# Gate and value of a gated layer as 2x2 block products by Strassen's algorithm, in two sweeps over the tokens

## What is computed

```python
def _moe_ref(x, w_in, w_out):
    h = x @ w_in                                   # 2304 x 512 by 512 x 2048
    g = np.where(h > 0.0, h, np.exp(np.minimum(h, 0.0)) - 1.0)
    return g @ w_out                               # back to 512
...
def _moe2_ref(x, w_gate, w_val, w_out):
    g = x @ w_gate                                 # 512 x 1536
    silu = g * (1.0 / (1.0 + np.exp(-g)))
    val = x @ w_val                                # 512 x 1536
    return silu * val @ w_out                      # 1536 x 512
```

## Time and profile before

| | |
|---|---|
| median of 3 runs | 999.63 us (999.11 to 1001.42) |
| the profiled execution | 999.19 us, of which the span of the trace is 997.3 |
| TensorE busy | 985.8 us, 99% of the span, 7040 matmuls |
| VectorE, ScalarE, GpSimd busy | 46%, 34%, 12% |
| second layers on TensorE | from 542.87 us to the end |

### The profile page before, as it was taken

How to read it: one execution, slowest core, us unless ns; L and a number is a source line. 1 busy time by engine, 2 the same in 40 slices (tenths; PEclk the granted TensorE clock), 3 DMA queues, 4 the chain that set the end, 5 groups by cost and what they waited for, 6 DMA issues and landing times.

```text
span 997.3 us, 17826 instructions
## 1 busy us (share of the span) xinstructions
PE 985.8 (99%) x7040; PEld 912.5 (91%) x7040; DVE 455.7 (46%) x1151; ACT 341.0 (34%) x953; POOL 115.0 (12%) x138
## 2 busy tenths in 40 slices
PE   8899999999999999999999999999999999999998
PEld 5889999999999999999999888888888888889997
DVE  7888755556555565564343332223222322322222
ACT  5565544444435344443346321212121221212112
POOL 7204510023000000000057500000000000000000
PEclk9999999999999999999999999999999999999999
DMA  8544521124102111110434300200020001001000
GB/s 241 184 123 106 104 52 43 45 60 100 33 26 77 42 38 33 58 30 1 154 120 131 116 1 1 76 1 1 1 77 1 1 29 47 1 1 39 1 1 37
DMA packets 45666, 55.68 MB, mean 56 GB/s; under 512 B 6504, under 2 KB 33992, under 8 KB 45584
## 3 DMA queue, kind: packets, MB, share of 16 engines
q1 hardware_dynamic: 38128, 50.61, 16.5%
q0 software_dynamic: 6816, 3.55, 2.6%
q10 hardware_dynamic: 640, 0.39, 0.2%
HBM read 45.08 MB, written 9.44 MB: 55 GB/s over the span
## 4 chain that ended last, share of the span: by engine, by line
PE 95%; DVE 2%; ACT 2%; DMA 1%; issue 0%; ACTq 0%; POOL 0%; DVEq 0%; POOLq 0%
PE bank L455 29%; PE bank L457 28%; PE bank L456 28%; PE bank L419 2%; PE bank L386 2%; PE bank L404 1%; PE bank L441 1%; PE bank L395 1%; ACT weights L785 1%; DMA q_first<-qT 1%; DVE weights L616 1%; PE bank L429 0%; ACT prob L746 0%; DVE g_sb L641 0%; ACTq L360 0%
## 5 line engine op out<-in xcount | busy, mean ns | idle before, releaser
L455 PE MATMUL bank<-x_hl,weights 128*128 128x464 f32 (+3 forms) x928 | 325.8, 351 | 4.0 <-DVE weights L616 2.8
L457 PE MATMUL bank<-x_hl,weights 128*128 128x464 f32 (+3 forms) x928 | 322.0, 347 | 0.0
L456 PE MATMUL bank<-x_hl,weights 128*128 128x464 f32 (+3 forms) x928 | 321.9, 347 | 0.0
L455 PEld LDWEIGHTS bank<-x_hl,weights 128*128 128x128 f32 x928 | 175.5, 189 | 15.3 <-DVE weights L616 3.9
L456 PEld LDWEIGHTS bank<-x_hl,weights 128*128 128x128 f32 x928 | 175.6, 189 | 10.2
L457 PEld LDWEIGHTS bank<-x_hl,weights 128*128 128x128 f32 x928 | 175.5, 189 | 10.3
L455 PE MATMUL bank<-g_hl,weights 128*128 128x384 f32 (+1 forms) x448 | 147.7, 330 | 0.0
L457 PE MATMUL bank<-g_hl,weights 128*128 128x384 f32 (+1 forms) x448 | 143.3, 320 | 0.0
L456 PE MATMUL bank<-g_hl,weights 128*128 128x384 f32 (+1 forms) x448 | 143.2, 320 | 0.0
L659 DVE TENSOR_TENSOR u_sb<-bank,u_sb 128x464 f32<-128x464 f32 (+1 forms) x60 | 38.3, 638 | 202.3 <-ACT u_sb L807 202.3
L807 ACT ACTIVATE u_sb<-bank 128x464 f32<-128x464 f32 (+1 forms) x60 | 33.3, 555 | 196.4 <-PE bank L457 196.4
(11 more groups left out here) (96 smaller groups left out, 1062.5 us busy)
## 6 DMA issues: line engine op xcount, KB each, us to landing
landing<-w SPq DMA_DIRECT2D x44, 256.0 KB, 4.0
v_win<-v_windows SPq DMA_DIRECT2D x46, 105.0 KB
q_sb<-qT SPq DMA_DIRECT2D x88, 48.0 KB, 2.3
k_sb<-kT SPq DMA_DIRECT2D x14, 288.0 KB, 3.7
yT_scratch<-y_sb SPq DMA_DIRECT2D x20, 192.0 KB, 2.0
y_raw<-yT_scratch SPq DMA_DIRECT2D x4, 928.0 KB, 5.3
outT<-out_sb SPq DMA_DIRECT2D x16, 232.0 KB, 2.3
landing<-wg SPq DMA_DIRECT2D x12, 256.0 KB, 2.9
```

The costliest lines, as they stand in the source:

```text
L455: nc.tensor.matmul(out, w_hi, x_hi, start=first, stop=False)
L456: nc.tensor.matmul(out, w_hi, x_lo, start=False, stop=False)
L457: return nc.tensor.matmul(out, w_lo, x_hi, start=False, stop=last)
```

## The change

The gate matrix and the value matrix are each seen as 2x2 blocks: 256 input features by 128 hidden columns a block. The input is seen as blocks of 256 features by 256 tokens. For a pair of column blocks and 512 tokens, the four result blocks are made from seven block products instead of eight (the Winograd form), for gate and for value side by side in one bank (2 x 256 columns). The products are named p1, u2, u3, u4, c11, c21, c12. They need sums of weight blocks (`dve_sum_weights`, 4 operations for each matrix and pair), sums of input blocks (`dve_sum_blocks`, 4 for a tile), and seven sums of results on the way out of PSUM: a copy of p1 on ScalarE, and `dve_u2`, `dve_u3`, `dve_c22_u4` (two), `dve_c11`, `dve_c21`, `dve_c12` on VectorE. Seven blocks instead of four are split into high and low parts.

Since seven weight blocks with their low parts do not fit for all 12 column blocks, the hidden columns are done in two sweeps of three pairs. A sweep visits all tokens: one narrow tile of 256 tokens, done by plain block products, and four wide ones of 512; the second sweep goes backwards. The narrow tile is first and last. A visit and a pair are an item: 30 items. The first sweep's partial result goes to a scratch in HBM (`partT`), and comes back in the second, where VectorE adds it (`dve_out`). The second sweep's weights are loaded, summed and split between items 13 and 18. GpSimd's low parts are instructions of 1024 and 768 columns instead of 512. TensorE's order around an item is five products, the accumulation of the item before, two products. There is one buffer for u in place of two. A product may take a bank when the sum of the product four turns before has been made (`take_bank`).

```diff
+BLOCK = 2 * P
+HALF2 = 256
+WIDE2 = 2 * HALF2
...
+PAIRS2 = NF2 // 2 // SWEEPS
...
+STARTS2 = [0] + [HALF2 + WIDE2 * t for t in range(NT2 - 1)]
+WIDTHS2 = [HALF2] + [WIDE2] * (NT2 - 1)
+assert STARTS2[-1] + WIDE2 == TOKENS
+VISITS = [(0, t) for t in range(NT2)] + [(1, t) for t in reversed(range(NT2))]
...
+XBUF = [0, 1, 0, 1, 0, 0, 1, 0, 1, 0]
...
...
+TURNS = [(n, x) for n, (v, _) in enumerate(ITEMS) for x in (PRODUCTS if is_wide(v) else (0, 1))]
...
+W_PARTS = [(0, 4), (4, 7)]
+W_OPS = 2 * len(W_PARTS) + 1
...
+                gv_hl.append(rw(f"gv_hl{p}_{j}", [P, 2, 7, BLOCK], F32R))
+            w3_raw.append(nc.alloc_sbuf_tensor_at(f"w3_raw{p}", [P, 2, PIECE], F32, offset=rw.at + 2 * PIECE * 4))
...
+        p1_sb = rw("p1_sb", [P, 2, HALF2], F32)
+        u2_sb = rw("u2_sb", [P, 2, HALF2], F32)
+        u3_sb = rw("u3_sb", [P, 2, HALF2], F32)
+        u4_sb = rw("u4_sb", [P, 2, HALF2], F32)
+        u_sb = rw("u_sb", [P, 2, WIDE2], F32)
+        u_hl = rw("u_hl", [P, 2, 2, WIDE2], F32R)
...
-        def pe_gate_val(pe, t, f):
...
-        def pe_accumulate2(pe, t, f):
...
+        def block_product(out, n, j, w, x, opens, closes):
+            v, p = ITEMS[n]
+            b, weight = XBUF[v], gv_hl[2 * p + j]
+            for c in range(2):
+                k, cols = slice(c * P, (c + 1) * P), slice(c * HALF2, (c + 1) * HALF2)
+                mm = three_passes(out, (weight[:, 0, w, k], weight[:, 1, w, k]), x2_hl[b][:, 0, x, cols],
+                                  x2_hl[b][:, 1, x, cols], opens and c == 0, closes and c == 1)
+            return mm
...
+        def take_bank(pe, n, x):
+            k = TURNS.index((n, x))
+            if k >= len(gv_banks):
+                m, y = TURNS[k - len(gv_banks)]
+                if is_wide(ITEMS[m][0]):
+                    pe.wait_ge(sum_done[y], wides(m) + 1)
+                else:
+                    pe.wait_ge(uv_done, 2 * m + y + 1)
+            return gv_banks[k % len(gv_banks)]
...
+        def pe_product(pe, n, x):
+            v, p = ITEMS[n]
+            bank = take_bank(pe, n, x)
+            w, b = PRODUCTS[x]
+            if p == 0:
+                pe.wait_ge(x2_lo_done, before_load(v, 4, 2) + X_NEEDS[b])
+            for j in range(2):
+                wait_weights(pe, v, p, 2 * (j + 1))
+                mm = block_product(bank[:, j * HALF2:(j + 1) * HALF2], n, j, w, b, True, True)
+            mm.then_inc(product_done[x], 1)
...
+        def pe_narrow(pe, n, f):
...
+            first, last = ((0, 0), (1, 1)) if f == 0 else ((4, 0), (3, 2))
+            for j in range(2):
+                wait_weights(pe, v, p, 2 * (j + 1))
+                out = bank[:, j * HALF2:(j + 1) * HALF2]
+                block_product(out, n, j, first[0], first[1], True, False)
+                mm = block_product(out, n, j, last[0], last[1], False, True)
+            mm.then_inc(narrow_done, 1)
...
+        def pe_accumulate2(pe, n):
+            v, p = ITEMS[n]
+            w = WIDTHS2[VISITS[v][1]]
...
+            pe.wait_ge(u_hi_done, 2 * n + 2)
+            pe.wait_ge(u_lo_done, 2 * n + 2)
...
             for m in range(KC):
...
+                if p == 0:
+                    pe.wait_ge(acc_free, KC * (NT1 + v - 1) + m + 1)
+                cols = slice(m * P, (m + 1) * P)
+                for f in order:
+                    mm = three_passes(acc[m][:, 0:w], (w3_hl[p][:, 0, f, cols], w3_hl[p][:, 1, f, cols]), u_hl[:, 0, f, 0:w],
+                                      u_hl[:, 1, f, 0:w], p == 0 and f == order[0], p == PAIRS2 - 1 and f == order[1])
+                if p == PAIRS2 - 1:
...
+            for n in range(-1, len(ITEMS)):
+                nxt = n + 1 if n + 1 < len(ITEMS) else None
+                if nxt is not None and not is_wide(ITEMS[nxt][0]):
+                    pe_narrow(pe, nxt, 0)
+                    pe_narrow(pe, nxt, 1)
+                elif nxt is not None:
+                    pe_product(pe, nxt, "p1")
+                    pe_product(pe, nxt, "u2")
+                    pe_product(pe, nxt, "u3")
+                    pe_product(pe, nxt, "u4")
+                    pe_product(pe, nxt, "c11")
+                if n >= 0:
+                    pe_accumulate2(pe, n)
+                if nxt is not None and is_wide(ITEMS[nxt][0]):
+                    pe_product(pe, nxt, "c21")
+                    pe_product(pe, nxt, "c12")
 
 
 
...
+        def dve_sum_weights(dve, h, p, j):
+            x, i = gv_raw[2 * p + j], 4 * (2 * (PAIRS2 * h + p) + j)
+            dve.wait_ge(gv_loaded[p][j], 16 * (h + 1))
+            nc.vector.tensor_tensor(x[:, 4, :], x[:, 2, :], x[:, 3, :], ALU.add).then_inc(gv_summed, 1)
+            dve.wait_ge(gv_summed, i + 1)
+            nc.vector.tensor_tensor(x[:, 2, :], x[:, 0, :], x[:, 2, :], ALU.subtract).then_inc(gv_summed, 1)
+            nc.vector.tensor_tensor(x[:, 5, :], x[:, 4, :], x[:, 0, :], ALU.subtract).then_inc(gv_summed, 1)
+            dve.wait_ge(gv_summed, i + 3)
+            nc.vector.tensor_tensor(x[:, 6, :], x[:, 1, :], x[:, 5, :], ALU.subtract).then_inc(gv_summed, 1)
...
+        def dve_sum_blocks(dve, v):
+            x, i = x_raw2[XBUF[v]], before_load(v, 4, 1)
+            dve.wait_ge(x2_loaded[XBUF[v]], x2_count(v))
...
+            nc.vector.tensor_tensor(x[:, 4, :], x[:, 2, :], x[:, 0, :], ALU.subtract).then_inc(x2_summed, 1)
+            dve.wait_ge(x2_summed, i + 1)
+            nc.vector.tensor_tensor(x[:, 2, :], x[:, 3, :], x[:, 2, :], ALU.subtract).then_inc(x2_summed, 1)
+            nc.vector.tensor_tensor(x[:, 5, :], x[:, 3, :], x[:, 4, :], ALU.subtract).then_inc(x2_summed, 1)
+            dve.wait_ge(x2_summed, i + 3)
...
+        def dve_blocks_low(dve, v):
+            b, i = XBUF[v], before_load(v, 4, 2)
+            for k, (lo, hi) in enumerate(x_parts(v)):
+                dve.wait_ge(x2_hi_done, i + k + 1)
+                nc.vector.tensor_tensor(x2_hl[b][:, 1, lo:hi, :], x_raw2[b][:, lo:hi, :], x2_hl[b][:, 0, lo:hi, :].bitcast(F32),
+                                        ALU.subtract).then_inc(x2_lo_done, 1)
...
+        def dve_u2(dve, n):
+            k = wides(n)
+            dve.wait_ge(product_done["u2"], k + 1)
+            dve.wait_ge(sum_done["p1"], k + 1)
+            nc.vector.tensor_tensor(u2_sb[:, :, :], of_bank(n, "u2"), p1_sb[:, :, :], ALU.add).then_inc(sum_done["u2"], 1)
...
+        def dve_c22_u4(dve, n):
+            k = wides(n)
+            dve.wait_ge(product_done["u4"], k + 1)
+            dve.wait_ge(sum_done["u3"], k + 1)
+            wait(dve, sg_done, 2 * n)
+            nc.vector.tensor_tensor(gv_sb[:, :, 1, HALF2:WIDE2], of_bank(n, "u4"), u3_sb[:, :, :], ALU.add).then_inc(c22_done, 1)
+            nc.vector.tensor_tensor(u4_sb[:, :, :], of_bank(n, "u4"), u2_sb[:, :, :], ALU.add).then_inc(sum_done["u4"], 1)
...
+        def dve_gate(dve, n, i):
...
+            dve.wait_ge(sg_done, 2 * n + i + 1)
+            nc.vector.tensor_tensor(u_sb[:, f, 0:w], g, u_sb[:, f, 0:w], ALU.mult).then_inc(gs_done, 1)
...
+            nc.vector.tensor_tensor(u_sb[:, f, 0:w], x, u_sb[:, f, 0:w], ALU.mult).then_inc(uv_done, 1)
...
+        def dve_out(dve, v):
...
+            dve.wait_ge(part_loaded, 16 * (v - NT2 + 1))
+            for m in range(KC):
+                dve.wait_ge(acc2_done, v * KC + m + 1)
+                nc.vector.tensor_tensor(out_sb[:, m, 0:w], acc[m][:, 0:w], out_sb[:, m, 0:w], ALU.add).then_inc(acc_free, 1)
...
-                        dve_swiglu(dve, t + 1, 0)
-                    if f == SPLIT_STEP and t + 1 < NT2:
-                        dve_split_y(dve, t + 1)
+                    dve_sum_blocks(dve, 0)
+                if s == FIRST_Y_SPLIT_STEP + 2:
+                    dve_blocks_low(dve, 0)
+            for n, (v, p) in enumerate(ITEMS):
+                if is_wide(v):
+                    dve_u2(dve, n)
+                    dve_u3(dve, n)
+                    dve_c22_u4(dve, n)
+                    dve_c11(dve, n)
+                    for h, q in sums_of(v, p):
+                        dve_sum_weights(dve, h, q, 0)
+                        dve_sum_weights(dve, h, q, 1)
+                    if p == 0 and v - 1 >= NT2:
+                        dve_out(dve, v - 1)
+                    if p == 1 and v + 1 in LOADED:
+                        dve_sum_blocks(dve, v + 1)
+                    if p == 2 and v + 1 in LOADED:
+                        dve_blocks_low(dve, v + 1)
+                    dve_c21(dve, n)
+                    dve_gate(dve, n, 0)
+                    dve_c12(dve, n)
...
+        def act_gv_high(act, h, p, j):
...
+            for lo, hi in W_PARTS:
+                nc.scalar.activation(gv_hl[2 * p + j][:, 0, lo:hi, :], gv_raw[2 * p + j][:, lo:hi, :], ACT.Copy).then_inc(w2_hi_done, 1)
...
+        def act_blocks_high(act, v):
...
+            for lo, hi in x_parts(v):
+                nc.scalar.activation(x2_hl[b][:, 0, lo:hi, :], x_raw2[b][:, lo:hi, :], ACT.Copy).then_inc(x2_hi_done, 1)
...
+        def act_p1(act, n):
```

(84 more changed lines are left out.)

358 lines of the change are left out of this document (214 added, 144 removed).

## The result

The changed kernel takes 1003.87 us (median of 20 runs, 1000.74 to 1011.69), the kernel before 999.32 (20 runs, 998.38 to 1003.01). The ratio is 1.0040 [1.0029, 1.0051]: 0.4% slower, where 991 us was forecast. The profiled execution took 1005.7 us, span 1003.9, 1.8 above its own median; the span before was 997.3.

What follows compares the result with a forecast made beforehand. TensorE was taken as the bound, through matmul count and the pitch between starts. -19.4 + 2 + 8.9 - 0.3 = -8.8 us on 999.19 (median 999.63) gave 991 us; range 979 to 1001, likeliest case 986 to 996.

Steps and rivals of the forecast that it cites:

- The matmuls, -19.4 us: Second layers on TensorE: 2448 matmuls of 256 columns at 122 ns and 576 of 512 at 231.2, 431.8 us against 451.2.
- Rival C: Chance 0.08: the weight load sets the pitch at 256 columns too; by the upper bound of 133.0 ns, 1011 us.
- The steady item, at nothing: Steady wide items, 15.80 us of TensorE: VectorE and ScalarE finish in time, with 0.8 and 2.1 us to spare; no cost.
- rival D: Chance 0.12: VectorE's and ScalarE's steady order misses the c11 bank; 0.7 us of wait per wide item gives 1007 us.
- the last tile of layer 1: Making sweep one's weights there adds 1.7 us of VectorE work a step, which fits; cost nothing, bound 3 us.
- Start, +2 us: Start of the second layers: visit 1's first low parts ready at 25.4 us, TensorE at 23.4; bounds 0 and 5.
- Change of weights, +8.9: Items 14 to 16: GpSimd's long instructions delay VectorE's gate and value chain, 2.7, 2.7 and 3.5 us; bounds 0 and 15.
- Rival B: Chance 0.20: the stalls do not come about, GpSimd's operations fall into other gaps; 982 us, or 978 at 120.2 ns.
- Ends, -0.3: End of the kernel: last low part due 2.9 us after its last product, chain 2.5; tail after the last matmul 0.3 shorter.
- The clock: Granted TensorE clock: not a term of the sum; only mentioned as possibly lowered by waits in every item.

Runs made afterwards that it cites:

- the fill of zeros: The changed kernel with GpSimd writing zeros as the low parts of the second layers' weights instead of subtracting, leaving them out of the computation: 985.65 us, 0.9859.
- two halves: The changed kernel with the narrow items' gated result in two halves of the u buffer in turn: 993.6 us, 0.9928.
- the fill of the pauses: The changed kernel with unused matmuls, 40 ahead of the first wide item and 24 ahead of the last third-matrix group: 1001.64 us, 1.0013.
- the best version: The changed kernel with u in halves, low parts of visit 1's input ahead of item 2's chain, and all weight low parts on VectorE, none on GpSimd: 977.62 us.

## Why the prediction was wrong

**The matmuls, -19.4 us: right, and too small.** The pitch at 256 columns is 119.9 ns, not 122; of the two ways of working it out, the line down from 384 through 464 (120.2) was the good one. At 512 columns it is 227.5 to 227.8 ns, not 231.2. Measured: -26.2. Rival C (133 ns, the weight load) is out.

**The steady item, at nothing: right.** 604.36 to 619.89 is 15.53 us (15.80 predicted) with no wait, though the cover was 0.8 us; rival D is out as a mechanism of the steady state. VectorE's share from 620 to 700 us is 69%, ScalarE's 28%, as forecast.

**"I cost that at nothing, bound 3 us" (the last tile of layer 1): the step that failed most.** It cost 7.8 us. I counted VectorE's own new work there, at 1.7 us a step, and found room for it. The count was short (3.4 us stand ahead of the low part at 536.11, with the low parts of visit 0's input), but there was room even so: with the fill of zeros the same six operations stand there and nothing stops. I left out what GpSimd's long instructions do to layer 1's chain, though the next part of the prediction reckons with just that effect in mid-course. The stalled operation, the ELU's L800, has one SBUF input, a form for which the earlier trace rows show nothing.

**Start, +2 us: mis-sized.** The pause was 5.83, above the bound of 5. I had "VectorE sums the blocks only behind item 1 (13.8 to 16.7)", but the wait of the high part on the single u buffer had pushed those sums to 17.6 to 20.3 after the start at 552.51, and item 2's chain likewise. With two halves the pause is 2.53, near the forecast.

**Change of weights, +8.9: right in mechanism and place.** Pauses of 2.35, 1.57 and 2.71, in sum 6.6, against 2.7, 2.7 and 3.5, released by ScalarE's p1 copy. Rival B, that the stalls do not come, is out.

**Ends, -0.3: half right.** After the last matmul -0.5. But the "2.9 us after its last product" in which the last low part was to be made was not there: same u buffer, +3.6.

**The clock: not in the sum.** Only rival D held it, as a consequence. It cost 7.3 us in the second layers and 1.3 in layer 1, since long pauses were followed by half-speed matmuls; the fill of the pauses shows the link. Each stall was priced as its own length.

In sum: -26.2 + 15.4 + 7.3 + 0.9 is -2.6 for the second layers, and +7.8 in layer 1, +1.8 between executions and -0.5 at the end make the span's +6.6 within rounding. The medians differ by 4.6. The sign was decided by two terms that I had at nothing, the last tile and the clock: without either, the medians would have come out lower. The pauses at the start and the end, 3.7 and 3.5 us above their terms, are about made up by the matmuls, 6.8 below theirs.

**What stays open.** Why the last 3.7 us of pauses in the best version stay was not tried. That the low clock is the whole of the spread of the changed kernel's runs is only argued, from their rows, which overlap: 1000.7 to 1004.6 us at a mean clock of 0.990 or 0.991, 1003.3 to 1006.1 at 0.985 to 0.988, 1011.7 at 0.980. Why the same pause is followed by a fall in one profile and not in another is open too.
